# Second layer's gate and value by seven block products in place of eight, with the sums of weights and of x formed on the chip

## The chip, the cores and the metric

One core of one Trainium2 chip runs the whole program. The metric is the device time of one execution in microseconds (us); the time before is the median of three runs.

## The reference, cut to what matters

```python
def _moe_ref(x, w_in, w_out, g_ln):                 # first layer, x: 2304 x 512
    h = x @ w_in                                    # 1024 hidden
    ...                                             # softmax times h, layer norm
    return (ln @ w_out).astype(np.float32)

def _moe2_ref(x, w_gate, w_val, w_out):             # second layer
    gate = 1.0 / (1.0 + np.exp(-(x @ w_gate)))      # 512 x 1536
    val = x @ w_val                                 # 512 x 1536
    return (gate * val @ w_out).astype(np.float32)  # 1536 x 512

def reference(**kwargs):
    attn_out = _attn_ref(**attn_kwargs)             # 4 batches, 8 heads, 576 rows, 64 wide
    ...
    x = _moe_ref(x=x, **moe_kwargs)
    return _moe2_ref(x=x, **moe2_kwargs)
```

## The kernel before, in words

The program has three stages: attention over 16 pairs of heads (from the fifth pair on mixed with the first layer's tiles), the rest of the first layer alone, and the second layer. 2304 tokens are 18 tiles of 128. x lies transposed in `xT` (four rows of 128 channels by 2304 tokens). All matrix products are made from pairs of a rounded high part (`_hi`, written by ScalarE, ACT) and the remainder (`_lo`, by VectorE, DVE, or GpSimd, POOL): three matmuls (hi hi, hi lo, lo hi) for each product.

**The tail of the first layer** (the loops `for i in range(t + 1, TILES)`, t = 11, in the blocks of tensor, vector and scalar). In iteration i TensorE (PE) turns the normalized tile i (L1086, 8 transposes), turns the output of tile i-1 (L1106), makes the hidden product of tile i+2 (L1076, 24 matmuls of 512 columns) and the output product of tile i (L1099, 24 more), which waits for `ln_lo_ok`. DVE in its own order: `moe_ln_low(i)` (L821, two instructions), `moe_store_x(i-1)` (L801), the maximum of tile i+2 (L777), its rows and statistics (L784 to L812, with two trips to ACT and one to POOL), and `moe_norm` (L814). For i = 16 and 17 there is no tile i+2: in its place PE makes the first two steps of the second layer (`gate_val(0, 0)` and `(0, 1)`). Meanwhile ACT and POOL split the first 384 tokens of x (L540, L447) and the first four weight blocks (L537, L442).

**The second layer** walks over 6 chunks of 384 tokens (`CH`) and, inside one, over 12 blocks f of 128 hidden columns (`FB2`): 72 steps. A step is `gate_val(c, f)` on PE: 12 matmuls 128x384 for the gate into one bank (L1199 to L1201, 4 channel blocks by 3), 12 for the value into another; then ACT takes the sigmoid (L552), DVE multiplies by the value (L902), ACT rounds (L559), DVE subtracts (L905), and PE adds the step before into the output with `out_block` (L1214 to L1216, 3 tiles by 3 matmuls of 512 columns). After f = 11 DVE moves the three output banks out (L935) through two buffers and SyncE's queue (SP) stores them (L396). The weights are loaded once (L380 to L382), split once and stay. At a chunk's start ACT (L540) and POOL (L447, x_lo) split the next 384 tokens of x. The chunks 1 to 5 are one hardware loop on PE.

The order of work is written out by hand: each engine runs its own list, and semaphores tie them.

## Time and profile before

| | |
|---|---|
| runs | 909.24, 910.42, 910.52 us, median 910.42 |
| profiled execution | 908.74 us, its span 907.0 us |
| PE busy | 875.7 us, 97% |
| DVE, ACT, POOL busy | 407.3, 351.8, 104.4 us |
| second layer alone, 465.6 us to the end | PE without a gap but for some tenths at a chunk's start |
| moved by DMA | 33.73 MB |

The profile is of one execution. Its trace gives the start and length of each instruction, and what ended the idle time before it. A matmul's length there holds its drain: successive matmuls overlap, so what one costs is read from start to start. The span leaves out 1.7 us of the execution's time.

### The profile page before, as it was taken

The numbers are of one execution on the slowest core, as the hardware profiler recorded it, in microseconds if no ns is written. First come the engines' busy times: TensorE is split into PE (matmuls) and PEld (weight loads), VectorE is DVE, ScalarE is ACT, GpSimd is POOL, SyncE is SP. The second block draws the span as 40 slices with busy tenths as digits, with TensorE's granted clock in tenths as the row PEclk, the third lists the DMA queues.
The fourth block names the chain that finished last, engine by engine and source line by source line (L and its number), as shares of the span: only waits on it lengthen the run. The fifth ranks groups of instructions, "written<-read, shape, count | busy, mean of one in ns | idle before, by whom it ended". The sixth has DMA issues, their size and how long they took to land.

```text
span 907.0 us, 14321 instructions
## 1 busy us (share of the span) xinstructions
PE 875.7 (97%) x5440; PEld 735.8 (81%) x5440; DVE 407.3 (45%) x1104; ACT 351.8 (39%) x772; POOL 104.4 (12%) x83
## 2 busy tenths in 40 slices
PE   5788899999999999999999999999999999999997
PEld 2555677777777778778899999999999999999996
DVE  5888876766666675355425121121121112112112
ACT  4777665656665653345443121121121112112111
POOL 1000000000000001135266010010010001001000
PEclk9999999999999999999999999999999999999999
DMA  5151111111111000400350000000000000000000
GB/s 186 44 173 44 41 42 42 42 39 32 39 42 42 16 16 14 140 1 4 101 169 6 1 36 1 1 35 0 0 35 0 0 0 35 0 0 35 0 0 35
DMA packets 36803, 33.73 MB, mean 37 GB/s; under 512 B 5776, under 2 KB 27280, under 8 KB 36752
## 3 DMA queue, kind: packets, MB, share of 16 engines
q1 hardware_dynamic: 36752, 33.06, 11.8%
q8 instruction: 31, 0.51, 0.2%
q14 instruction: 20, 0.16, 0.1%
HBM read 28.33 MB, written 4.72 MB: 36 GB/s over the span
## 4 chain that ended last, share of the span: by engine, by line
PE 93%; DVE 4%; issue 1%; ACT 1%; DMA 1%; SPq 0%; POOL 0%; DVEq 0%; ACTq 0%
PE m_bk L1076 9%; PE s_bk L1099 7%; PE tt_bk L1199 6%; PE s_bk L1201 6%; PE s_bk L1199 6%; PE s_bk L1200 6%; PE tt_bk L1201 5%; PE tt_bk L1200 5%; PE o_bk L1099 4%; PE s_bk L965 4%; PE tt_bk L1013 4%; PE o_bk L1021 4%; PE m_bk L1216 4%; PE m_bk L1215 4%; PE m_bk L1214 4%; PE s_bk L1076 2%
## 5 line engine op out<-in xcount | busy, mean ns | idle before, releaser
L902 DVE TENSOR_TENSOR gv<-gv,s_bk 128x384 f32<-128x384 f32 x71 | 39.3, 554 | 279.7 <-PE s_bk L1201 279.7
L483 ACT ACTIVATE p_nat<-p_nat,negmax 128x512 f32<-128x512 f32 (+2 forms) x144 | 83.0, 578 | 75.0 <-DVE negmax L716 75.0
L552 ACT ACTIVATE gv<-tt_bk 128x384 f32<-128x384 f32 x70 | 34.5, 492 | 198.7 <-PE tt_bk L1201 198.7
L559 ACT CAST gv_hi<-gv 128x384 fp32r<-128x384 f32 x72 | 36.9, 513 | 156.6 <-PE m_bk L1216 135.9
L1199 PE MATMUL s_bk<-x_hi,w_hi 128*128 128x384 f32 x288 | 96.3, 334 | 0.0
L1201 PE MATMUL s_bk<-x_hi,w_lo 128*128 128x384 f32 x288 | 96.2, 334 | 0.0
L1200 PE MATMUL s_bk<-x_lo,w_hi 128*128 128x384 f32 x288 | 96.2, 334 | 0.0
L1199 PE MATMUL tt_bk<-x_hi,w_hi 128*128 128x384 f32 x280 | 94.8, 338 | 0.1
L1201 PE MATMUL tt_bk<-x_hi,w_lo 128*128 128x384 f32 x280 | 94.4, 337 | 0.0
L1200 PE MATMUL tt_bk<-x_lo,w_hi 128*128 128x384 f32 x280 | 94.0, 336 | 0.0
L905 DVE TENSOR_TENSOR gv_lo<-gv,gv_hi 128x384 fp32r<-128x384 f32 x72 | 51.9, 721 | 46.4 <-ACT gv_hi L559 46.4
L716 DVE CUSTOM_DVE_ANT_0 p_nat<-s_bk,mask 128x512 f32<-128x512 f32 (+3 forms) x128 | 56.5, 487 | 27.0 <-PE s_bk L965 26.8
L1013 PE MATMUL tt_bk<-ident,p_nat 128*128 128x128 f32 x400 | 56.2, 278 | 10.3 <-DVE memo L754 6.2
L1013 PEld LDWEIGHTS tt_bk<-ident,p_nat 128*128 128x128 f32 x400 | 47.1, 143 | 22.5 <-issue 16.4
L447 POOL TENSOR_TENSOR x_lo<-xT,x_hi 128x384 fp32r<-128x384 f32 x24 | 23.8, 1015 | 310.9 <-ACT x_hi L540 310.7
L965 PE MATMUL s_bk<-qkT 64*64 64x256 f32 (+3 forms) x512 | 49.6, 482 | 10.3 <-DVE negmax L716 5.7
L1216 PE MATMUL m_bk<-w_hi,gv_lo 128*128 128x512 f32 x144 | 57.1, 397 | 0.0
L1215 PE MATMUL m_bk<-w_lo,gv_hi 128*128 128x512 f32 x144 | 56.8, 395 | 0.0
L490 ACT COPY pT<-tt_bk 128x512 f32<-128x512 f32 (+1 forms) x80 | 43.1, 559 | 35.3 <-PE tt_bk L1013 33.7
L1214 PE MATMUL m_bk<-w_hi,gv_hi 128*128 128x512 f32 x144 | 56.6, 393 | 0.0
L1199 PEld LDWEIGHTS tt_bk<-x_hi,w_hi 128*128 128x128 f32 x280 | 52.6, 188 | 4.5 <-POOL x_lo L447 1.7
L1200 PEld LDWEIGHTS tt_bk<-x_lo,w_hi 128*128 128x128 f32 x280 | 52.6, 188 | 2.8
(142 smaller groups left out, 1757.5 us busy)
## 6 DMA issues: line engine op xcount, KB each, us to landing
qkT<-in_q SPq DMA_DIRECT2D x16, 288.0 KB, 2.8
qkT<-in_k SPq DMA_DIRECT2D x16, 288.0 KB, 3.2
out<-o_sb SPq DMA_DIRECT2D x18, 256.0 KB, 2.0
v_raw<-in_v SPq DMA_DIRECT2D x16, 256.0 KB, 2.7
w_raw<-in_moe_w_gate SPq DMA_DIRECT2D x12, 256.0 KB, 4.7
w_raw<-in_moe_w_val SPq DMA_DIRECT2D x12, 256.0 KB, 4.9
w_raw<-in_moe_w_out SPq DMA_DIRECT2D x12, 256.0 KB, 5.7
xT<-in_moe_w_in SPq DMA_DIRECT2D x1, 2048.0 KB, 8.5
```

Source lines behind the costliest of these rows:

```text
L483: nc.scalar.activation(p_tile(g, tile), p_tile(g, tile), ACT.Exp, bias=negmax[:, n:n + 1], scale=-1.0, accum_out=den[:, n:n + 1]).then_inc ...
L716: last = nc.vector.tensor_tensor_reduce(out=to, in0=s_tile(tile), in1=m, scale=-SCALE, scalar=3.0e38, op0=ALU.add, op1=ALU.min, accum_out= ...
L965: last = mm(s_tile(tile)[c * D:c * D + D, :], qkT[r, g % 2, 0, a:a + D], qkT[r, g % 2, 1, 0:keys(tile)], start=True, stop=True, skip_group ...
L1013: last = nc.tensor.transpose(bank[:, c * P:(c + 1) * P], p_nat[g % 2][:, p_at[tile] + j * P:p_at[tile] + (j + 1) * P], ident[:, :])
L1076: last = mm(h_banks(even)[:, n, :], x[:, b, :], w[:, b, c], start=m % (3 * DC) == 0, stop=m % (3 * DC) == 3 * DC - 1)
L1099: last = mm(y_bank(tail), ln[:, f * P:(f + 1) * P], w[:, f, :], start=m == 0, stop=m == 3 * FB - 1)
L1199: mm(o, w3_hi[f][:, a], x2_hi[:, d, :], start=d == 0, stop=False)
L1200: mm(o, w3_hi[f][:, a], x2_lo[:, d, :], start=False, stop=False)
L1201: last = mm(o, w3_lo[f][:, a], x2_hi[:, d, :], start=False, stop=d == DC - 1)
L1214: mm(o, gv_hi[b][:, t], w3_hi[f][:, w], start=f == 0, stop=False)
L1215: mm(o, gv_hi[b][:, t], w3_lo[f][:, w], start=False, stop=False)
L1216: last = mm(o, gv_lo[b][:, t], w3_hi[f][:, w], start=False, stop=f == FB2 - 1)
```

## The change

The 2304 tokens are now walked in 3 groups of 768 (two halves a and b of 384), with 12 blocks f each: 36 steps n. One step's gate and value for both halves are a product of a 2 by 2 block matrix of weights (rows gate and value, columns the two halves of the 512 channels) with a 2 by 2 block matrix of x (the halves of the channels, the halves a and b). It is made from seven block products (6 matmuls 128x384 each, two channel blocks by three):

- S1 = A21+A22, S2 = S1-A11, S3 = A11-A21, S4 = A12-S2 of the weights (A11, A12 gate; A21, A22 value), by DVE `add_w` in every step;
- T1 = B12-B11, T3 = B22-B12, T2 = B22-T1, T4 = B21-T2 of x, by DVE `add_x`, once a group;
- PE adds A11 B11, S2 T2, S1 T1, S4 B22 in this order into one bank (the chain), A12 B21, then S3 T3 and A22 T4 into the second (the side). Between them ACT copies the running sums out (`keep_p1`, `keep_u2`, `keep_u4`), and DVE adds the side to them (`gate_a`, `val_b`, `val_a`). So PE waits within a step for `p1_ok`, `gate_a_ok`, `u2_ok`, `u4_ok`, `val_b_ok`, and at the next for `sig_b_ok` and `val_a_ok`.

The six output tiles of the step before are put between the products. The gate's and value's weights are loaded and split anew in all 36 steps through three raw buffers; only the output weights stay. Their splitting and that of x goes from POOL to DVE. The loops are written out in full. The last three tiles leave through buffers of their own.

```diff
-            def split_w3(f):
-                pool.wait_ge(w3_hi_ok, f + 1)
...
-            with pool.Fori(1, CHUNKS) as c:
-                for b in range(DC):
-                    split_x2_block(c, b)
...
             def load_w3(f):
...
+                sp.dma_start(w3_raw[f][:, :], w3o_v[:, f, :]).then_inc(w3_in[f], 16)
+
+            def load_wc(n):
+                f, r = n % FB2, wc_raw[n % NR]
+                wait(sp, wc_lo_ok, 2 * (n - NR + 1))
...
             sp.wait_ge(x_ok, 2 * PAIRS)
+            load_wc(0)
+            for f in range(2):
                 load_w3(f)
             sp.wait_ge(h_ready, TILES)
+            for n in range(1, NR + 1):
+                load_wc(n)
+            sp.wait_ge(yt_ready, TILES)
+            for f in range(2, FB2):
                 load_w3(f)
...
+            for n in range(NR + 1, STEPS):
+                load_wc(n)
+                if n % FB2 == 4 and n > FB2:
+                    store_b(n // FB2 - 1)
+                    store_a(n // FB2 - 1)
```

ScalarE's list of one step (`leaves`: last f of a group, `enters`: first f of the next):

```diff
+            def pair_step(n):
...
+                keep_p1(n)
+                if leaves:
+                    split_xc(p + 1, B11)
+                sig_a(n)
+                if leaves:
+                    split_xc(p + 1, B21)
+                if enters:
+                    split_xc(p, B22)
+                keep_u2(n)
+                if enters:
+                    split_xc(p, T4)
+                if n + 1 < STEPS:
+                    split_wc(n + 1, 0)
+                    split_wc(n + 1, 1)
+                keep_u4(n)
+                if 1 < n < FB2:
+                    split_w3(n)
+                if enters:
+                    evacuate_b(p - 1)
...
+                sig_b(n)
...
+                keep_hi_b(n)
```

VectorE's list of one step, and what it does in the first layer's tail:

```diff
+            def pair_step(n):
...
+                gate_a(n)
...
+                if f == 1 and p:
+                    evacuate_a(p - 1)
+                if n == 0:
+                    add_w(1)
+                if n + 2 < STEPS and n and not enters:
+                    add_w(n + 2)
...
+                if n + 1 < STEPS:
+                    low_wc(n + 1, 0)
...
+                val_b(n)
+                if n + 1 < STEPS:
+                    low_wc(n + 1, 1)
+                if n == 0 or enters:
+                    add_w(n + 2)
+                if 1 < n < FB2:
+                    low_w3(n)
+                if 4 <= f < 8 and p < GROUPS - 1:
+                    add_x(p + 1, (T1, T3, T2, T4)[f - 4])
...
+                times_b(n)
+                val_a(n)
+                low_b(n)
+                times_a(n)
...
+                low_a(n)
...
+                if i == t + 1:
+                    dve.wait_ge(yt_ok, 2 * CT)
+                    dve.wait_ge(x_ok, 2 * PAIRS)
+                    add_x(0, T1)
+                    add_x(0, T3)
+                    add_x(0, T2)
+                    add_x(0, T4)
+                elif i == t + 2:
+                    low_xc(0, B11)
+                    low_xc(0, B21)
+                    low_xc(0, T2)
+                    low_xc(0, T3)
+                elif i == t + 3:
+                    add_w(0)
+                    low_xc(0, T1)
+                    low_xc(0, B22)
+                    low_xc(0, T4)
+                elif i == t + 4:
+                    low_w3(0)
+                    low_wc(0, 0)
+                    low_wc(0, 1)
```

TensorE's list of one step (`between(k)` is one output tile, or in steps 0 and 1 four matmuls of the first layer's output product):

```diff
+            def products(n, between):
...
+                product(n, B11, True).then_inc(chain_ready, 1)
...
+                product(n, B21, True).then_inc(side_ready, 1)
+                between(0)
...
+                pe.wait_ge(p1_ok, n + 1)
+                product(n, T2, False).then_inc(chain_ready, 1)
+                pe.wait_ge(gate_a_ok, n + 1)
+                product(n, T3, True).then_inc(side_ready, 1)
+                between(1)
+                pe.wait_ge(u2_ok, n + 1)
+                product(n, T1, False).then_inc(chain_ready, 1)
+                between(2)
+                between(3)
+                pe.wait_ge(u4_ok, n + 1)
+                product(n, B22, False).then_inc(chain_ready, 1)
+                pe.wait_ge(val_b_ok, n + 1)
+                product(n, T4, False).then_inc(side_ready, 1)
+                between(4)
+                between(5)
...
-            with pe.Fori(1, CHUNKS) as c:
-                chunk(c)
+            for n in range(2, STEPS):
+                products(n, lambda k, n=n: out_tile(n - 1, k))
+            for k in range(2 * CT):
+                out_tile(STEPS - 1, k)
```

**DVE in the first layer's tail.** Before, in iteration 14 of the tail, the norm of tile 16 (L814) is followed at once by the remainder of tile 15 (L821), for which PE's output product waits:

```order
L812 TENSOR_SCALAR st<-st 128x1
L814 TENSOR_SCALAR u_even<-u_even,st 128x1024 [waits ln_b]
L821 TENSOR_TENSOR ln_lo<-tt_bk,ln_hi 128x512 [waits ln_hi_ok] x2
L801 TENSOR_SCALAR xT<-s_bk 128x4x128 [waits yt_ready]
L777 TENSOR_REDUCE st<-m_bk 128x1 [waits h_ready]
```

Now the same place (L954 is the norm, L961 the remainder, L1062 to L1067 `add_w`, L1054 `low_xc`):

```order
L954 TENSOR_SCALAR u_even<-u_even,st 128x1024 [waits ln_b]
L1062 TENSOR_TENSOR wc_raw0<-wc_raw0 128x256 [waits wc_in0]
L1063 TENSOR_TENSOR wc_raw0<-wc_raw0 128x256
L1065 TENSOR_TENSOR wc_raw0<-wc_raw0 128x256 [waits s1_ok]
L1067 TENSOR_TENSOR wc_raw0<-wc_raw0 128x256 [waits s2_ok]
L1054 TENSOR_TENSOR xc_lo<-xc_raw,xc_hi 128x768 [waits xc_hi_ok]
L1054 TENSOR_TENSOR xc_lo<-xT,xc_hi 128x768 [waits xc_hi_ok]
L1054 TENSOR_TENSOR xc_lo<-xc_raw,xc_hi 128x768 [waits xc_hi_ok]
L961 TENSOR_TENSOR ln_lo<-tt_bk,ln_hi 128x512 [waits ln_hi_ok] x2
L941 TENSOR_SCALAR xT<-s_bk 128x4x128 [waits yt_ready]
```

Seven instructions of DVE have moved in ahead of the remainder; iterations 12, 13 and 15 have four, four and three such.

**SP's queue after the first layer.** Before (L380 gate, L381 value, L382 output weights of a block; from the wait on, five blocks of three rows):

```order
L380 DMA w_raw<-in_moe_w_gate 128x4x128
L381 DMA w_raw<-in_moe_w_val 128x4x128
L382 DMA w_raw<-in_moe_w_out 128x512
L380 DMA w_raw<-in_moe_w_gate 128x4x128 [waits yt_ready]
L381 DMA w_raw<-in_moe_w_val 128x4x128
L382 DMA w_raw<-in_moe_w_out 128x512
```

Now (L445 an output weight block, L450 and L452 value and gate of a step; the pair behind the ten blocks is `load_wc(4)`):

```order
L450 DMA wc_raw<-in_moe_w_val 128x4x128 [waits wc_lo_ok]
L452 DMA wc_raw<-in_moe_w_gate 128x4x128
L445 DMA w_raw<-in_moe_w_out 128x512 [waits yt_ready]
L445 DMA w_raw<-in_moe_w_out 128x512 x9
L450 DMA wc_raw<-in_moe_w_val 128x4x128 [waits wc_lo_ok]
L452 DMA wc_raw<-in_moe_w_gate 128x4x128
```

`load_wc(4)` stands behind ten transfers that wait for the last tile of the first layer; before, the first blocks behind that wait were those of steps 7 to 11.

## Rows read from the trace of the kernel before

**Rows 1.** The page, parts 1 and 2: PE's busy time; its granted clock in 40 slices

```profile
PE 875.7 (97%) x5440; PEld 735.8 (81%) x5440; DVE 407.3 (45%) x1104; ACT 351.8 (39%) x772; POOL 104.4 (12%) x83
...
PEclk9999999999999999999999999999999999999999
```

**Rows 2.** Busy time by stretch (stretch: length, busy us per engine, clock), second layer

```profile
600.00:700.00 100.00, 99.97 (x527) 93.26 (x527) 20.50 (x36) 17.75 (x36) 5.29 (x6) 1.00 0.04 16
```

**Rows 3.** Timeline (start, length, engine, line, operation): one step on PE

```profile
641.70 0.33 PE L1199 MATMUL tt_bk<-x_hi,w_hi 128*128 128x384 f32 x1
...
643.80 0.33 PE L1199 MATMUL s_bk<-x_hi,w_hi 128*128 128x384 f32 x1
...
645.88 0.39 PE L1214 MATMUL m_bk<-w_hi,gv_hi 128*128 128x512 f32 x1
...
647.96 0.33 PE L1199 MATMUL tt_bk<-x_hi,w_hi 128*128 128x384 f32 x1
```

**Rows 4.** Timeline of PE: the fourth step's (f = 3) first matmul

```profile
465.56 0.33 PE L1199 MATMUL tt_bk<-x_hi,w_hi 128*128 128x384 f32 x1
```

**Rows 5.** Timeline: the end, last matmul and last copy

```profile
901.62 0.40 PE L1216 MATMUL o_bk<-w_hi,gv_lo 128*128 128x512 f32 x1
903.64 0.69 DVE L935 COPY o_sb<-o_bk 128x512 f32<-128x512 f32 x1 [1.50 <-DMA out<-o_sb]
```

**Rows 6.** Groups by line and shape, DVE: subtractions of 384 (from 500 us on), 1024

```profile
L905 DVE TENSOR_TENSOR gv_lo<-gv,gv_hi 128x384 fp32r<-128x384 f32 x64 | 35.8, 560 | 40.8 <-ACT gv_hi L559 40.8
...
L766 DVE TENSOR_TENSOR w_lo<-xT,w_hi 128x1024 fp32r<-128x1024 f32 x4 | 4.9, 1216 | 0.0
```

**Rows 7.** Timeline of ACT: roundings of 384 and of 1536 columns

```profile
397.74 0.51 ACT L540 CAST x_hi<-xT 128x384 fp32r<-128x384 f32 x1
398.15 1.48 ACT L537 CAST w_hi<-w_raw 128x1536 fp32r<-128x1536 f32 x1
```

**Rows 8.** Timeline of DVE in the first layer's tail

```profile
389.25 0.81 DVE L814 TENSOR_SCALAR u_moe<-u_moe,st 128x1024 f32<-128x1024 f32 x1
...
400.15 1.29 DVE L821 TENSOR_TENSOR ln_lo<-tt_bk,ln_hi 128x512 fp32r<-128x512 f32 x2 [0.26 <-ACT ln_hi L528]
401.36 0.68 DVE L801 TENSOR_SCALAR xT<-s_bk 128x512 f32<-128x512 f32 x1
404.15 1.22 DVE L777 TENSOR_REDUCE st<-m_bk 128x1 f32<-128x1024 f32 x1 [2.12 <-PE m_bk L1076]
...
410.98 1.41 DVE L814 TENSOR_SCALAR u_moe<-u_moe,st 128x1024 f32<-128x1024 f32 x1
...
435.93 1.42 DVE L814 TENSOR_SCALAR u_moe<-u_moe,st 128x1024 f32<-128x1024 f32 x1
```

**Rows 9.** Timeline of PE there: output products of tiles 13 and 14; step 0

```profile
403.95 0.40 PE L1099 MATMUL o_bk<-w_hi,ln_hi 128*128 128x512 f32 x1
...
416.43 0.40 PE L1099 MATMUL o_bk<-w_hi,ln_hi 128*128 128x512 f32 x1
...
435.81 0.42 PE L1199 MATMUL s_bk<-x_hi,w_hi 128*128 128x384 f32 x1
```

**Rows 10.** Timeline of POOL there: the split of x

```profile
410.82 1.02 POOL L447 TENSOR_TENSOR x_lo<-xT,x_hi 128x384 fp32r<-128x384 f32 x1 [0.25 <-ACT x_hi L540]
```

**Rows 11.** Timeline of SP's queue, and busy time by stretch (last number GB/s)

```profile
461.62 0.37 SPq L380 DMA_DIRECT2D w_raw<-in_moe_w_gate  x1
...
471.84 1.25 SPq L382 DMA_DIRECT2D w_raw<-in_moe_w_out  x1
...
476.00:478.00 2.00, 2.00 (x11) 1.65 (x10) 1.14 (x2) 0.51 (x1) 1.93 (x1) 1.00 0.22 77
```

**Rows 12.** Busy time by stretch (granted clock third from the end), early attention

```profile
24.00:26.00 2.00, 1.10 (x7) 0.83 (x7) 0.68 (x4) 1.91 (x6) 0.00 (x0) 0.87 0.06 10
26.00:28.00 2.00, 1.80 (x8) 1.35 (x7) 1.24 (x5) 0.73 (x3) 0.00 (x0) 0.50 0.03 8
28.00:30.00 2.00, 1.87 (x13) 1.19 (x12) 1.94 (x3) 1.58 (x6) 0.00 (x0) 0.78 0.00 0
```

More of the change, by code:

```diff
@@ L82, in attn_moe_kernel @@
     T_END = PAIRS - M0
+    A22, A11, A12, S1, S2, S3, S4 = range(7)
+    B11, B21, T2, T3, T1, B22, T4 = range(7)
+    W_OF = (A11, A12, S2, S3, S1, S4, A22)
+    SIDE = (0, 1, 0, 1, 0, 0, 1)
+    STEPS = GROUPS * FB2
+    OUT_TILES = (3, 4, 5, 0, 1, 2)
     with ExitStack() as ctx:
@@ L389, in _ @@
+            sp.wait_ge(yt_ready, TILES)
+            for f in range(2, FB2):
                 load_w3(f)
[L390 to L401 removed]
@@ new lines, in split_xc @@
+            def split_xc(p, j):
+                if p:
+                    n = p * FB2 - 1
+                    if SIDE[j]:
+                        act.wait_ge(side_ready, 3 * n + (B21, T3, T4).index(j) + 1)
+                    else:
+                        act.wait_ge(chain_ready, 4 * n + (B11, T2, T1, B22).index(j) + 1)
+                if j in (T1, T2, T3, T4):
+                    act.wait_ge(xs_ok, 4 * p + (T1, T3, T2, T4).index(j) + 1)
+                elif p == 0:
+                    act.wait_ge(yt_ok, 2 * CT)
+                nc.scalar.copy(xc_hi[:, j, :, :], x_sum(p, j)).then_inc(xc_hi_ok, 1)
@@ new lines, in keep_p1, with sig_a, keep_u2 @@
+            def keep_p1(n):
+                act.wait_ge(chain_ready, 4 * n + 1)
+                nc.scalar.copy(c_p1[:, :], pair_banks(n)[0]).then_inc(p1_ok, 1)
+            def sig_a(n):
+                act.wait_ge(gate_a_ok, n + 1)
+                wait(act, lo_a_ok, n)
+                nc.scalar.activation(gv_a[:, :], c_p1[:, :], ACT.Sigmoid).then_inc(sig_a_ok, 1)
+            def keep_u2(n):
+                act.wait_ge(chain_ready, 4 * n + 2)
+                wait(act, gv_a_ok, n)
+                nc.scalar.copy(c_u2[:, :], pair_banks(n)[0]).then_inc(u2_ok, 1)
@@ new lines, in keep_u4, with sig_b, keep_hi_b @@
+            def keep_u4(n):
+                act.wait_ge(chain_ready, 4 * n + 3)
+                wait(act, gv_b_ok, n)
+                nc.scalar.copy(c_u4[:, :], pair_banks(n)[0]).then_inc(u4_ok, 1)
+            def sig_b(n):
+                act.wait_ge(chain_ready, 4 * n + 4)
+                wait(act, lo_b_ok, n)
+                nc.scalar.activation(gv_b[:, :], pair_banks(n)[0], ACT.Sigmoid).then_inc(sig_b_ok, 1)
+            def keep_hi_b(n):
+                act.wait_ge(gv_b_ok, n + 1)
+                wait(act, out_ready, 2 * CT * (n - 2) + CT if n > 1 else 0)
+                nc.scalar.copy(gv_hi[1][n % 2][:, :], gv_b[:, :]).then_inc(hi_b_ok, 1)
@@ new lines, in pair_step @@
+            def pair_step(n):
+                p, f = n // FB2, n % FB2
+                enters, leaves = f == 0 and p > 0, f == FB2 - 1 and p < GROUPS - 1
+                gate_a(n)
+                if leaves:
+                    low_xc(p + 1, B11)
+                if enters:
+                    low_xc(p, T1)
+                    low_xc(p, B22)
+                if f == 1 and p:
[4 more added lines that the diff above has]
+                    add_w(n + 2)
+                if leaves:
+                    low_xc(p + 1, B21)
+                if n + 1 < STEPS:
+                    low_wc(n + 1, 0)
+                if enters:
+                    low_xc(p, T4)
+                val_b(n)
[7 more added lines that the diff above has]
+                    add_x(p + 1, (T1, T3, T2, T4)[f - 4])
+                if leaves:
+                    low_xc(p + 1, T2)
+                times_b(n)
+                val_a(n)
+                low_b(n)
+                times_a(n)
+                if leaves:
+                    low_xc(p + 1, T3)
+                low_a(n)
```

487 lines of the change are left out of this document (293 added, 194 removed).

## The prediction

> **What bounds the kernel now.** I read the page first: PE is busy 97% of the span at full clock [rows 1]. Then the busy times by stretch: in the second layer PE is busy 99.97 of 100 us, DVE 20.5 and ACT 17.8 [rows 2]. Then the timeline of one step on PE. The gate takes 643.80-641.70 = 2.10 us, the value 2.08, the output block 2.08, and the next step follows at once: 6.26 us in all [rows 3]. So a matmul of 384 columns costs 2.08/12 = 0.173 us, one of 512 columns 2.08/9 = 0.231, and the first product behind an output block some 0.02 more. From 465.56 [rows 4] PE runs to 901.62+0.23 = 901.85 [rows 5], 436.3 us. The work in it, 69 gates and values of 4.18 and 70 output blocks of 2.08, is 434.0; the other 2.3 us are the starts of five chunks. PE's columns are the limit, so fewer of them are worth their time wherever PE needn't wait for something new.
>
> **What is removed.** Per block f and 768 tokens there were 48 matmuls of 384 columns, now 42; the 18 of 512 stay. Two old steps take 12.52 us. A new one: 42 x 0.173 = 7.28, 18 x 0.231 = 4.16, four returns from an output tile to a product 0.08, together 11.52. Over 36 steps **-36.0**. The chunk starts go with the chunks: **-2.3**; what stands in their place is costed below. At the end, 907.0-901.85 = 5.15 us lie behind PE, since the third copy had to wait for a store [rows 5]. Now each last tile has its own buffer: 0.1 + copy 0.69 + store (907.0-903.64-0.69 = 2.67) = 3.5. **-1.7**. The gain without any new wait is 40.0.
>
> **The steady step, by its queues.** Prices: two-input DVE instructions of 384 columns 0.56, of 1024 1.22 [rows 6], so by the line between them 256 take 0.43 and 768 0.95 (0.08 less from start to start). ACT roundings: 384 take 0.51, 1536 1.48 [rows 7], so 768 0.83 and 1024 1.05. DVE has per step 7 of 384 (3.9), `add_w` 4 x 0.43 = 1.7 with its own waits, `low_wc` 0.95+1.22: 7.8 us of 11.5. ACT has 7 x 0.5 + 0.83 + 1.05 = 5.4. Neither binds by its sum. By order, from the step's start: B11 ends at 1.04, B21 2.08, T2 runs 2.77 to 3.81, T3 to 4.85, T1 5.54 to 6.58, B22 7.97 to 9.01, T4 to 10.05 (about 0.2 more until a result may be read).
> - `keep_p1` 1.2 to 1.75 is in time for T2 at 2.77. `gate_a` 2.3 to 2.9 is in time for T3 at 3.81.
> - `keep_u2` 4.0 to 4.5, for T1 at 5.54. Behind it on ACT the two splits end at 6.4, so `keep_u4` runs 6.8 to 7.3, for B22 at 7.97: the tightest, 0.65 us over.
> - `val_b` 7.3 to 7.9 for T4 at 9.01. `sig_b` and `times_b` end at 10.3, `val_a` 10.9, for B21 of the next step at 12.56. `low_a` ends at 1.7 of the next step, before `gate_a`.
> In steps 4 to 11 `low_w3` (0.7) and an `add_x` (0.95) stand ahead of `times_b`, which comes at 10.7: still in time. I take no wait; `add_w`, `low_wc` and the splits are hidden under PE's products, and if that cover fails they cost what rival 4 prices. The reload of 512 KB per step is hidden too: a buffer comes free some 17 us before it is wanted, and transfers have landed within the 14.9 us that 15 of them took [rows 11].
>
> **The first layer's tail: +7.2.** Here DVE's additions stand ahead of what PE waits for. Before, the remainder of tile 13 (L821) ends at 401.44 and PE wants it at 403.95: 2.5 us of slack [rows 8, 9]. The old splits on POOL go, which had held the norm at 1.41 us while POOL split x [rows 8, 10]; alone it takes 0.81, so 0.6 comes back in each iteration.
> - Iteration 12: four `add_x`, 3.6 us, less 2.5 and 0.6, is 0.5. But ACT's split of T2 waits for the third sum and holds its own rounding of tile 13: 0.8.
> - From then on DVE is the longer ring: maximum to norm's end 412.39-404.15 = 8.24, less 0.6, then the addition, the remainder 1.45, the store of x 0.6: 9.7 plus the addition, against PE's 12.48 (416.43-403.95). Iteration 13 adds four `low_xc`, 3.6: +0.8. Iteration 14 adds `add_w(0)` 1.7 and three `low_xc` 2.65: +1.5.
> - Step 0 on PE was due at 435.81, now 438.9. It waits for `low_wc(0, 0)`. The norm of tile 17 ended at 437.35; now 0.6 sooner and 3.4 later, at 440.15, then `low_w3(0)` and `low_wc(0, 0)` until 441.7: +2.85.
> - The remainder of tile 16 behind `low_wc(0, 1)`: +0.4. In iteration 17 the turn of tile 16's output waits for ACT, whose copy now stands behind both halves of step 0: +0.8.
> Sum 7.15. Ends: 0, if the idle time of DVE took it all, and 14, which is all that DVE is given there (14.4).
>
> **Step 2: +3.8.** Step 2 starts where 465.56 was, plus 2.0 (twelve matmuls more are due by then) plus 7.2: 474.8; the last tile of x is turned at 472.0. That frees ten output-weight transfers, and `load_wc(4)` stands behind them. Before, 15 transfers of 256 KB took from 461.62 to about 476.5 [rows 11]. Twelve then take 11.9 and some 0.6 to be seen: 484.5. DVE comes to `add_w(4)` at 477.7 and sits; behind it are `low_wc(3, 0)` and `val_b(2)`, which end at 487.6. PE wants `val_b` at 474.8+9.0 = 483.8. Ends: 0 and 8 (if the transfers of 512-byte rows at the end go at half the rate). The Trainium skill, in "DMA: Bandwidth & Descriptors", section "Anatomy of one DMA", gives a fit of 2.0 us plus bytes by 436 GB/s, measured on another path. By it the twelve would be there after 9.2 us, the wait would be 0.5 and the sum 3.3 us lower; the rows of this queue (3.93 MB in 14.9 us, 264 GB/s) speak against it.
>
> **Group entries: +2.** In steps 11, 12 and 13 DVE gets seven `low_xc` and three copies, ACT seven splits and three copies. By the same lists `keep_u4(12)` is 0.2 late and `gate_a(13)` 0.1 to 0.3; with latencies 1 us for each of two entries. Ends 0 and 3 each, the latter if one list goes wholly late.
>
> **Sum.** 907.0-40.0+7.2+3.8+2.0 = 880.0 for the span, 1.7 more for the profiled execution (908.74 before), and the median before lies 1.7 over that execution (910.42): **883.5**.
>
> **Rivals.**
> 1. Nearly smooth: DVE's idle time takes the tail's additions and the queue keeps up. For it: DVE idles 2.1 us before each maximum [rows 8]. Against it: the additions stand behind the norm, not in that gap. Losses of 3: 873.5.
> 2. The clock falls. In early attention, in a stretch where PE was busy 1.10 of 2 us and then again little, the granted clock went to 0.87, 0.50 and 0.78 in three slices, so down to 1.2 GHz, which cost (0.13+0.50+0.22) x 2 = 1.7 us [rows 12]. The waits of 2.85 at step 0 and 3.8 at step 2 are such idle times: +3.4, 887. The Trainium skill, "TensorE: Matmul & The Clock Gate", section on the clock gate, makes the slow clock the default that only sustained work lifts; by it both waits would be followed by slow matmuls, and the trace agrees for attention.
> 3. A heavy start: DVE's and ACT's lists in the tail hold each other up (as T2's split does) to the upper end, and step 2 waits its 8: losses of 25, 895.
> 4. Slower: the ring between PE, ACT and DVE binds in each step. Place: `keep_u4` behind both splits on ACT, then `val_b`. It decides from 0.65 us of lateness there; to use up the 26.9 us, all of 34 steps must wait 0.8, so the two splits and the copy must take 1.45 more than 2.4. Each further 0.3 costs 10 us: 920 at 2.0. For it: five waits a step that were not there. Against it: every price comes from rows of the same shape, and DVE and ACT are quiet [rows 2].
>
> **How the numbers follow.** My sum 0.45, rival 1 0.13, rival 2 0.2, rival 3 0.14, rival 4 0.08 (a little of it not slower). About 0.2% (1.8 us) is what a measurement of this kernel can tell from none. Faster 0.92, within 0.2% 0.02, slower 0.06. Range: 873 to 898 leaves out the far part of rivals 1 and 3 and most of 4.
>
> **What would show it.** In the profile after: PE's period in steps 14 to 22 is 11.5 us, and PE waits there for nothing; if it is above 12, rival 4. PE waits for L961's remainder in iterations 13 to 15, some 3 us, and for L1073 before its first product of the second layer. In step 2 one wait of 3 to 5 us for L1089, DVE itself idle at L1062 on the DMA. The granted clock after these two waits tells rival 2. The last matmul is 3.5 us before the end. I am wrong in the main if the second layer's steps are not even, or if PE's matmul of 384 columns no longer goes at 0.173.

## The result, and the profile after

The changed kernel takes **880.54 us** (median of four runs, 878.8 to 883.05) against 910.42: ratio 0.9674, 95% interval 0.9659 to 0.969. The forecast was 883.5, the range 873 to 898. The profiled execution took 881.66 us, its span 879.7.

PE stays the bound, with 96% of a shorter span. DVE and ACT took over work: in the second layer DVE is now busy 70.7 of 100 us and ACT 47.1, where before it was 20.5 and 17.8 [rows 2]. From the page and the busy times by stretch (stretch: length, busy us of PE, PEld (its weight loads), DVE, ACT, POOL with counts, granted clock, DMA share, GB/s) of the changed kernel:

```profile
PE 842.2 (96%) x5224; PEld 700.8 (80%) x5224; DVE 601.7 (68%) x1464; ACT 464.2 (53%) x958; POOL 38.2 (4%) x47
...
600.00:700.00 100.00, 100.00 (x522) 92.86 (x521) 70.71 (x124) 47.11 (x83) 0.00 (x0) 1.00 0.20 63
```

The first matmuls of three steps in PE's timeline (start, length) give the period: 653.57 - 642.07 = 11.50 us, and over the steps 3 to 11 it is 11.48 or 11.49. The step that enters the second group (from 595.96) is hardly longer: the three steps around it take 11.52, 11.53 and 11.58.

```profile
595.96 0.33 PE L1449 MATMUL tt_bk<-xc_hi,wc_hi 128*128 128x384 f32 x1
...
642.07 0.34 PE L1449 MATMUL tt_bk<-xc_hi,wc_hi 128*128 128x384 f32 x1
...
653.57 0.34 PE L1449 MATMUL tt_bk<-xc_hi,wc_hi 128*128 128x384 f32 x1
```

**The tail**, to be held against [rows 8, 9]: the norm alone takes 0.81, four additions of 0.95 (the last two start 1.0 apart) stand ahead of the remainder L961, and PE waits behind it (the last bracket of a row is the idle time before it and what ended it).

```profile
400.30 0.81 DVE L954 TENSOR_SCALAR u_even<-u_even,st 128x1024 f32<-128x1024 f32 x1
401.03 0.95 DVE L1042 TENSOR_TENSOR xc_raw<-xT 128x768 f32<-128x768 f32 x1
...
405.10 1.29 DVE L961 TENSOR_TENSOR ln_lo<-tt_bk,ln_hi 128x512 fp32r<-128x512 f32 x2 [0.39 <-ACT ln_hi L596]
```

```profile
406.49 0.48 PE L1356 MATMUL o_bk<-w_hi,ln_hi 128*128 128x512 f32 x1 [0.67 <-issue]
...
442.35 0.41 PE L1449 MATMUL s_bk<-xc_hi,wc_hi 128*128 128x384 f32 x1 [2.36 <-issue]
```

**Step 2**, in three timelines. SP issues ten output-weight blocks and then the two transfers of `load_wc(4)`; DVE stands at L1062 until the second of them has landed, 7.74 us; PE stands behind DVE's L1089, 4.26 us.

```profile
472.32 5.85 SPq L445 DMA_DIRECT2D w_raw<-in_moe_w_out  x10
478.22 0.43 SPq L450 DMA_DIRECT2D wc_raw<-in_moe_w_val  x1
478.69 0.51 SPq L452 DMA_DIRECT2D wc_raw<-in_moe_w_gate  x1
479.24 0.73 SPq L450 DMA_DIRECT2D wc_raw<-in_moe_w_val  x1
```

```profile
485.53 0.42 DVE L1062 TENSOR_TENSOR wc_raw<-wc_raw 128x256 f32<-128x256 f32 x1 [7.74 <-DMA wc_raw<-in_moe_w_gate]
...
487.87 0.55 DVE L1089 TENSOR_TENSOR c_u<-c_u,tt_bk 128x384 f32<-128x384 f32 x1
```

```profile
488.47 0.44 PE L1449 MATMUL tt_bk<-xc_hi,wc_hi 128*128 128x384 f32 x1 [4.26 <-DVE c_u L1089]
```

Behind that wait the granted clock (third number from the end) falls. The burst of transfers starts slowly, at 76 and 177 GB/s in its first two slices; ahead of PE's wait the DMA engines are full (share 0.99 and more) at 318 to 353 GB/s.

```profile
472.00:474.00 2.00, 2.00 (x12) 1.65 (x11) 0.69 (x1) 0.00 (x0) 0.00 (x0) 1.00 0.31 76
474.00:476.00 2.00, 2.00 (x12) 1.82 (x11) 0.00 (x0) 0.00 (x0) 0.00 (x0) 1.00 0.63 177
...
480.00:482.00 2.00, 2.00 (x12) 1.82 (x11) 0.00 (x0) 1.36 (x3) 0.00 (x0) 1.00 0.99 318
482.00:484.00 2.00, 2.00 (x12) 1.67 (x10) 0.00 (x0) 0.80 (x2) 0.00 (x0) 1.00 1.11 353
...
488.00:490.00 2.00, 1.53 (x6) 1.53 (x7) 2.00 (x3) 0.00 (x0) 0.00 (x0) 0.76 0.00 0
490.00:492.00 2.00, 2.00 (x6) 1.61 (x6) 1.89 (x5) 0.51 (x1) 0.00 (x0) 0.50 0.56 168
492.00:494.00 2.00, 2.00 (x11) 1.86 (x11) 0.79 (x2) 0.69 (x2) 0.00 (x0) 0.88 0.32 94
```

**The end**, PE's and DVE's timelines, against [rows 5]: 879.7 - 876.23 = 3.5 us behind the last matmul, where 5.15 lay.

```profile
876.00 0.39 PE L1502 MATMUL s_bk<-w_hi,gv_loa 128*128 128x512 f32 x1
```

```profile
876.43 0.69 DVE L1123 COPY wc_raw<-s_bk 128x512 f32<-128x512 f32 x1
```

**How executions are compared.** The two spans differ by 27.3 us, but attention, whose code is the same, ended 1.7 us later in this execution: the hidden product behind it starts at 386.92, before at 385.21. So each trace is also read from that product to the end of its span, and called its rest: 907.0 - 385.21 = 521.8 us before, 879.7 - 386.92 = 492.8 after. The difference is 29.0. All twelve runs by both measures, each ratio against runs of the kernel before on the same chip. The variants ran on several chips, so two of them are compared by their ratios, not by their medians:

| kernel | time, us (runs) | ratio, interval | hidden product at | rest, us |
|---|---|---|---|---|
| before | 910.42 (4) | 1 | 385.21 | 521.8 |
| changed | 880.54 (4) | 0.9674, 0.9659 to 0.969 | 386.92 | 492.8 |
| e5_again, the same | 880.67 (5) | 0.9676, 0.9662 to 0.9689 | 385.84 | 492.7 |
| e1_queue | 877.06 (5) | 0.9636, 0.9619 to 0.9654 | 385.64 | 486.9 |
| e2_eight | 878.85 (5) | 0.9657, 0.9639 to 0.9675 | 386.94 | 491.5 |
| e3_slots | 881.34 (5) | 0.9676, 0.9654 to 0.9698 | 386.83 | 492.5 |
| e4_both | 875.68 (5) | 0.9614, 0.9598 to 0.9629 | 387.01 | 486.9 |
| e6_slots2 | 879.72 (5) | 0.966, 0.9647 to 0.9673 | 388.00 | 489.5 |
| e7_both2 | 873.16 (5) | 0.9584, 0.957 to 0.9599 | 386.76 | 484.4 |
| e9_best | 872.27 (5) | 0.9587, 0.9574 to 0.96 | 386.82 | 483.4 |
| e8_eighth | 917.8 (1) | none | 388.18 | 527.6 |
| e10_act2 | 883.18 (2) | 0.9703, 0.9685 to 0.9722 | 385.66 | 494.9 |
| e11_act4 | 895.8 (2) | 0.9842, 0.9823 to 0.9861 | 388.05 | 506.6 |
| e12_dve2 | 882.42 (2) | 0.9695, 0.9676 to 0.9714 | 386.70 | 492.9 |

### The profile page after: what moved, and what is told of

It reads as the page before. It is cut to its first block, busy times and chain, and to the rows that moved or that the text cites. A ratio compares the mean times of both kernels' runs of the same rounds, so it can differ in the third digit from the quotient of the medians.

```text
span 879.7 us, 14380 instructions
## 1 busy us (share of the span) xinstructions
PE 842.2 (96%) x5224; PEld 700.8 (80%) x5224; DVE 601.7 (68%) x1464; ACT 464.2 (53%) x958; POOL 38.2 (4%) x47
## 4 chain that ended last, share of the span: by engine, by line
PE 90%; DVE 5%; issue 2%; DMA 1%; ACT 1%; SPq 1%; POOL 0%; DVEq 0%; ACTq 0%
PE m_bk L1333 10%; PE tt_bk L1449 9%; PE tt_bk L1451 9%; PE tt_bk L1450 9%; PE s_bk L1356 7%; PE tt_bk L1270 5%; PE s_bk L1222 4%; PE o_bk L1356 4%; PE o_bk L1278 4%; PE s_bk L1501 3%; PE s_bk L1500 3%; PE s_bk L1502 3%; PE s_bk L1250 2%; PE s_bk L1333 2%; PE m_bk L1501 2%
## 5 line engine op out<-in xcount | busy, mean ns | idle before, releaser
L1449 PE MATMUL tt_bk<-xc_hi,wc_hi 128*128 128x384 f32 x476 | 160.1, 336 | 4.3 <-DVE c_u L1089 4.3
L1451 PE MATMUL tt_bk<-xc_hi,wc_lo 128*128 128x384 f32 x476 | 160.2, 337 | 0.0
L1450 PE MATMUL tt_bk<-xc_lo,wc_hi 128*128 128x384 f32 x476 | 160.0, 336 | 0.0
L1073 DVE TENSOR_TENSOR wc_lo<-wc_raw,wc_hi 128x768 fp32r<-128x768 f32 x72 | 78.3, 1088 | 30.8 <-ACT wc_hi L616 30.8
L1449 PEld LDWEIGHTS tt_bk<-xc_hi,wc_hi 128*128 128x128 f32 x476 | 89.5, 188 | 10.8 <-DVE c_u L1089 4.6
L1450 PEld LDWEIGHTS tt_bk<-xc_lo,wc_hi 128*128 128x128 f32 x476 | 89.5, 188 | 6.1
L1451 PEld LDWEIGHTS tt_bk<-xc_hi,wc_lo 128*128 128x128 f32 x476 | 89.5, 188 | 0.0
L616 ACT CAST wc_hi<-wc_raw 128x768 fp32r<-128x768 f32 x72 | 64.5, 945 | 1.8 <-DVE wc_raw L1067 1.8
L1333 PE MATMUL m_bk<-w_hi,x_hi 128*128 128x512 f32 x120 | 50.3, 419 | 1.5 <-issue 1.3
L880 DVE TENSOR_SCALAR p_nat<-p_nat,c_loc 128x512 f32<-128x512 f32 (+2 forms) x144 | 49.1, 398 | 1.7
L1333 PE MATMUL m_bk<-w_hi,x_lo 128*128 128x512 f32 x120 | 47.1, 393 | 0.0
L1089 DVE TENSOR_TENSOR c_u<-c_u,tt_bk 128x384 f32<-128x384 f32 x34 | 18.8, 554 | 36.1 <-ACT c_u L648 36.1
```

Of the source, the lines that this page charges most:

```text
L616: nc.scalar.copy(wc_hi[n % 2][:, k, :, :], wc_raw[n % NR][:, r, :, :]).then_inc(wc_hi_ok, 1)
L880: nc.vector.tensor_scalar(p, p, c_loc[:, t:t + 1], None, ALU.mult).then_inc(p_ok, 1)
L1073: nc.vector.tensor_tensor(wc_lo[n % 2][:, k, :, :], wc_raw[n % NR][:, r, :, :], wc_hi[n % 2][:, k, :, :].bitcast(F32), ALU.subtract).then_ ...
L1333: last = mm(h_banks(even)[:, n, :], x[:, b, :], w[:, b, c], start=m % (3 * DC) == 0, stop=m % (3 * DC) == 3 * DC - 1)
L1449: mm(o, hi[:, k, c, :], xc_hi[:, j, c, :], start=start and c == 0, stop=False, skip_group_check=True)
L1450: mm(o, hi[:, k, c, :], xc_lo[:, j, c, :], start=False, stop=False, skip_group_check=True)
```

## The experiments

### Do PE's columns set the period?

**e8_eighth**: one more block product in each step.

```diff
-                product(n, B22, False).then_inc(chain_ready, 1)
+                product(n, B22, False)
+                product(n, B22, False).then_inc(chain_ready, 1)
```

> Edit: TensorE makes the product S4 B22 twice in each step (eight block products in place of seven, nothing else), so the gate of half b holds it twice. My theory (TensorE's columns set the period: 6 matmuls of 0.173 us more): the period goes from 11.49 to 12.53 us, the time rises by 37.4 us to about 918. Rival (the period of 11.49 is set by the ring through ScalarE and VectorE, with TensorE's columns close below it): less than 30 us.

The period became 12.53 us (+1.04, six matmuls at 0.173), and a stretch of 100 us is full with matmuls again. (Its output is not the reference's, since the product is added twice.) The rest grew by 34.8 us. 36 x 1.04 = 37.4; the remaining -2.6 lie in step 2, where the wait was 3.17 in place of 4.26 and the clock did not fall (below). So a product of six matmuls costs just what it occupies on PE, and -36 for the removed ones is no accident. It is one execution, but the 1.04 us stand in each of its steady steps.

### How near are the other engines?

**e10_act2** and **e11_act4**: two and four more copies on ACT ahead of `keep_u4`.

```diff
+                if n > 1:
+                    for k in range(4):
+                        wait(act, pad_ok, 4 * (n - 2) + k - 1)
+                        nc.scalar.copy((pad0, pad1)[k % 2][:, 0:CH], c_p1[:, :]).then_inc(pad_ok, 1)
                 keep_u4(n)
```

> Edit: the changed kernel with two more ScalarE copies of 384 columns ahead of keep_u4 in steps 2 to 35. In a steady step of the profile ScalarE idles 0.62 us before keep_u4, and the copy is over 0.71 us before the product B22 that waits for it: 1.33 us, less some 0.1 for the semaphore. My theory: two copies (0.9 us) are hidden, period 11.49 us, hidden product to end 492.8 us. Rival (the period is already set by this ring): +0.9 us a step, +30 us.

> Edit: four such copies (1.7 to 1.8 us). My theory (the ring of TensorE and ScalarE binds from 1.2 us of addition on): 0.5 to 0.6 us of them show in each of 34 steps, period 12.0 to 12.1, +17 to +20 us (time 898 to 901), with TensorE waiting for keep_u4 before B22 in every step. Rival (more hidden, since what is late in one step is taken up in the next): under 5 us.

With two copies the period stays at 11.49; only the steps that enter a group take 0.5 and 0.3 more. The rest grew by 2.2, of which 1.3 are a fall of the clock in step 0 (below) and 0.8 these entries. With four the period is 11.85 to 11.94, 0.36 to 0.45 over, and the steps that enter a group take 13.27 and 12.67; the rest grew by 13.8, less than the 17 expected. In ACT's timeline of one step of e11_act4 (and PE's below it) the four copies come without a gap, then `keep_u4`, then B22:

```profile
643.37 1.75 ACT L693 COPY pad<-c_p 128x384 f32<-128x384 f32 x4
...
645.03 0.47 ACT L649 COPY c_u<-tt_bk 128x384 f32<-128x384 f32 x1
```

```profile
645.55 0.45 PE L1454 MATMUL tt_bk<-xc_hi,wc_hi 128*128 128x384 f32 x1
```

`keep_u4` starts 645.03-643.37 = 1.66 us behind the first copy. Of those 1.66 some 0.4 show, so about 1.3 are hidden. That agrees with the changed kernel's own rows (ACT's, then PE's): ACT idles 0.62 us before `keep_u4`, and the copy's end, 648.90+0.48 = 649.38, is 0.71 ahead of the B22 product at 650.09.

```profile
648.90 0.48 ACT L648 COPY c_u<-tt_bk 128x384 f32<-128x384 f32 x1 [0.62 <-PE tt_bk L1451]
```

```profile
650.09 0.33 PE L1449 MATMUL tt_bk<-xc_hi,wc_hi 128*128 128x384 f32 x1
```

**e12_dve2**: two more additions on DVE in steps 4 to 35.

```diff
                     add_w(n + 2)
+                if 3 < n:
+                    nc.vector.tensor_tensor(pad1[:, :], w3_lo[2][:, :].bitcast(F32),
+                                            w3_lo[2][:, :].bitcast(F32), ALU.add)
+                    nc.vector.tensor_tensor(pad0[:, 0:CH], w3_lo[2][:, 0:CH].bitcast(F32),
+                                            w3_lo[2][:, 0:CH].bitcast(F32), ALU.add)
```

> Edit: the changed kernel with two more VectorE additions (512 and 384 columns, some 1.1 us) behind add_w(n+2) in steps 4 to 35. VectorE idles 0.97 us before low_wc(n+1, 0) and 1.17 before val_b. My theory: hidden, period 11.49, no change (492.8 us from hidden product to end), but some tenths in the steps that enter a group. Rival (VectorE, busy 71 of 100 us in the second layer, is the bound behind TensorE): +1.1 us in 32 steps, +35 us.

Hidden: period 11.49, rest 492.9, with 0.1 and 0.4 us in the two steps at the first group entry. DVE is now busy 79.4 of 100 us there, and PE doesn't notice. Rival 4 (the ring binds) is out: on ACT about 1.3 us of work find room in a steady step, on DVE at least the 1.1 tried here.

### The wait in step 2

**e1_queue**: step 4's weights are asked for before the ten output-weight blocks.

```diff
-            for n in range(1, NR + 1):
+            for n in range(1, NR + 2):
                 load_wc(n)
...
-            for n in range(NR + 1, STEPS):
+            for n in range(NR + 2, STEPS):
                 load_wc(n)
```

> Edit: the weights of step 4 are asked for right after those of step 3, ahead of the ten output-weight transfers. My theory (step 2 waits because its VectorE list stands at add_w(4) for a transfer that is queued behind those ten; the fallen clock after it is the wait's consequence): TensorE's wait of 4.3 us for L1089 goes, the granted clock stays at 1.00 from 485 to 495 us, step 2 takes 11.5 us in place of 17.6, and the time falls by 6 us to about 874.5. Rival (the transfers are only moved: the ten output-weight blocks land later, so low_w3(2) and the output products of step 2 or 3 wait in its place): steps 2 to 4 together lose 3 us or more, 877 to 880. Rival (the clock falls there for another reason than the wait): slices below 1.00 remain near 490 us, 876.3.

What the theory said of step 2 holds to a tenth; both rivals are out. SP issues the pair of L450 and L452 at 450.98, DVE goes through L1062 without a wait, step 2 takes 485.20-473.66 = 11.54 us and step 3 11.59 (no loss moved there), and the clock is 1.00 throughout. From the trace of this variant, PE's timeline, DVE's timeline, and the busy times where the wait had been:

```profile
473.66 0.34 PE L1449 MATMUL tt_bk<-xc_hi,wc_hi 128*128 128x384 f32 x1
...
485.20 0.34 PE L1449 MATMUL tt_bk<-xc_hi,wc_hi 128*128 128x384 f32 x1
```

```profile
476.44 0.42 DVE L1062 TENSOR_TENSOR wc_raw<-wc_raw 128x256 f32<-128x256 f32 x1
```

```profile
484.00:488.00 4.00, 4.00 (x21) 3.64 (x21) 2.63 (x6) 1.51 (x3) 0.00 (x0) 1.00 0.43 129
```

The rest fell by 5.9 us, the 6 of the theory, but the median is 877.06 and not 874.5. By the ratios the gain is (0.9674 - 0.9636) x 910 = 3.5 us, and the intervals of the two ratios allow some 2 more or less. The same edit on the two variants with other places gives (0.9676 - 0.9614) x 910 = 5.6 and (0.966 - 0.9584) x 910 = 6.9. The three average 5.3.

**e2_eight**: step 4's weights after eight of the ten blocks.

```diff
-            for f in range(2, FB2):
+            for f in range(2, 10):
                 load_w3(f)
+            load_wc(NR + 1)
+            for f in range(10, FB2):
+                load_w3(f)
```

> Edit: the weights of step 4 are asked for after eight of the ten output-weight transfers. My theory (twelve transfers of 256 KB took some 13 us, about 1 us each, and what stands ahead in the queue is what is waited for): they land some 2 us sooner, TensorE's wait in step 2 falls from 4.3 to about 2.3 us. The clock tells how long a wait it bears: it fell behind 4.3 us and not behind 2.36 us at step 0. If it stays at 1.00 behind 2.3 us, the time falls by 2.0+1.8 = 3.8 us to 876.7; if any such wait in step 2 lets it fall, by 2.0 to 878.5.

The wait is 2.99 us, 1.3 shorter and not 2, and the clock falls as before; the rest is 1.3 lower. DVE goes through L1062 1.3 us sooner. SP issues the pair at 477.12 and 477.60, then the last two blocks and step 5's pair. The packets say in which order they move: a step's weights go in packets of 512 bytes, 1024 for a pair, and an output-weight block in packets of 2 KB. The DMA view of this variant counts, from 472 to 481, 481 to 483, 483 to 484 and 484 to 487.5 us:

```profile
DMA packets 1148, 2.09 MB, mean 232 GB/s; under 512 B 118, under 2 KB 142, under 8 KB 1147
DMA packets 1090, 0.65 MB, mean 325 GB/s; under 512 B 41, under 2 KB 1017, under 8 KB 1090
DMA packets 226, 0.37 MB, mean 372 GB/s; under 512 B 19, under 2 KB 53, under 8 KB 226
DMA packets 1089, 0.58 MB, mean 165 GB/s; under 512 B 46, under 2 KB 1060, under 8 KB 1089
```

Of 512 bytes ("under 2 KB" less "under 512 B") these are 24, 976, 34 and 1014. So step 4's pair moves mostly between 481 and 483, the last two blocks mostly behind it, and step 5's pair last: the order of issue, with an overlap of under 1 us. That what is issued behind a transfer slows it is not shown. What was mispriced is the block: at the 318 to 353 GB/s of the full slices 256 KB take 0.74 to 0.82 us, and 1 us is the mean with the slow start. Two blocks are then 1.5 to 1.6 us; why the gain is 1.3 stays open.

### The tail

**e3_slots**: the same additions and remainders, in places where DVE was thought idle (the three lists of an iteration: before the maximum, before the rows, before the variance; a fourth, from e6_slots2 on, behind the norm).

```diff
+            SLOTS = {
+                t + 1: ([(first_sum, 0, T1), (add_x, 0, T3)], [(add_x, 0, T2)], [(add_x, 0, T4)]),
+                t + 2: ([(low_xc, 0, B11), (low_xc, 0, B21)], [(low_xc, 0, T2)], [(add_w, 0)]),
+                t + 3: ([(low_xc, 0, T3), (low_xc, 0, T1)], [(low_xc, 0, B22)], [(low_xc, 0, T4)]),
+                t + 4: ([(low_w3, 0), (low_wc, 0, 0)], [(low_wc, 0, 1)], []),
+            }
```

> Edit: in the first layer's tail VectorE does the same additions and remainders of the second layer's operands, but in its idle places (before the maximum of tile i+2, before its rows, before its variance) and not behind the norm, ahead of the remainder that TensorE waits for. My theory (the 5.6 us that the tail takes longer come from the place of the additions, since VectorE idles 2 us before each maximum and in its trips to ScalarE): the tail costs 0 to 1.5 us, step 0 starts 50.6 to 52 us after the hidden product at 386.9 in place of 55.4, and the time falls by 4 to 5 us to about 876. Rival (VectorE's ring is full by its sum, and the place doesn't matter): the maximum or the rows come later by as much, the tail keeps its 5 us, 880.

No gain: step 0 starts 442.49-386.83 = 55.7 us behind the hidden product (55.4 in the changed kernel). The rival (a full ring, so the place doesn't matter) seems right by the time, and for iteration 12 it is. There DVE has no idle time before the maximum, and the first addition runs beside POOL's work in 1.98 us in place of 0.95; the maximum comes 2.8 us later, and PE waits 2.70 for a copy of ACT behind it. Behind that wait the granted clock falls as well, (0.30+0.50+0.05) x 2 = 1.7 us in three slices: from the output product of tile 12 to that of tile 13 PE takes 409.92-392.97 = 16.95 us, where it took 12.59 before the change, 4.4 more. POOL's, DVE's and PE's timelines of this variant, and its busy times by stretch:

```profile
393.26 1.29 POOL L509 TENSOR_TENSOR x_lo<-xT,x_hi 128x512 fp32r<-128x512 f32 x1 [2.81 <-ACT x_hi L579]
```

```profile
393.38 1.98 DVE L1042 TENSOR_TENSOR xc_raw<-xT 128x768 f32<-128x768 f32 x1
395.29 0.94 DVE L1044 TENSOR_TENSOR xc_raw<-xT 128x768 f32<-128x768 f32 x1
396.15 1.21 DVE L917 TENSOR_REDUCE st<-s_bk 128x1 f32<-128x1024 f32 x1
```

```profile
402.37 0.41 PE L1362 MATMUL s_bk<-ident,y_nat 128*128 128x128 f32 x2 [2.70 <-ACT y_nat L601]
```

```profile
402.00:404.00 2.00, 1.63 (x7) 1.47 (x8) 1.15 (x3) 2.00 (x4) 0.55 (x1) 0.70 0.03 8
404.00:406.00 2.00, 2.00 (x6) 1.52 (x6) 1.06 (x2) 1.40 (x3) 0.00 (x0) 0.50 0.00 0
406.00:408.00 2.00, 2.00 (x10) 1.62 (x9) 2.00 (x4) 0.00 (x0) 0.00 (x0) 0.95 0.00 0
```

From iteration 13 on the loss was gone but for 0.6 us in iteration 14 (where PE waits 0.47 for ACT's copy): step 0 starts 442.49-435.58 = 6.91 us behind the output product of tile 15, as before the change (435.81-428.90), where the changed kernel takes 9.62.

**e4_both**: this with the queue's edit.

> Edit: both the earlier request for step 4's weights and the additions in VectorE's idle places. My theory (the two losses are separate, one ring in the first layer's tail, one queue in step 2): the gains add, 6+5 = 11 us, about 869.5, and TensorE waits for nothing of note from 387 us on. Rival (they are not separate: a tail that ends 5 us sooner wants the transfers of the queue 5 us sooner): less than the sum, 872 to 875.

Rest 486.9, the same as the queue's edit alone: one gain of 5.9 and one of nothing add. The 11 us of the theory needed the gain that e3_slots didn't bring, so its rival is not decided here. Iteration 12 lost the same here, a wait of 2.70 and a fallen clock behind it.

**e6_slots2**: nothing before the maximum in iteration 12 (the diff is against e3_slots; ACT's splits of T2 and T4 come one iteration later too).

```diff
-                t + 1: ([(first_sum, 0, T1), (add_x, 0, T3)], [(add_x, 0, T2)], [(add_x, 0, T4)]),
+                t + 1: ([], [(first_sum, 0, T1)], [(add_x, 0, T3)], []),
+                t + 2: ([(add_x, 0, T2), (low_xc, 0, B11)], [(add_x, 0, T4)], [(low_xc, 0, B21)], []),
...
+                t + 4: ([(low_xc, 0, B22), (low_xc, 0, T4)], [(low_w3, 0)], [(low_wc, 0, 0)], [(low_wc, 0, 1)]),
```

> Edit: VectorE's additions in its idle places, but none before the maximum in iteration 12, where it has no idle time (there the trace of the first such variant shows the additions ending 2.8 us after the maximum could begin, and TensorE waiting 2.70 us for the copy that ScalarE makes behind it); two of the four sums of x move to iteration 13, and ScalarE's split of T2 with them. My theory (the loss of the tail is where the additions stand): step 0 starts 50.6 to 51.6 us after the hidden product in place of 55.4, the time from hidden product to end falls from 492.8 to about 488.4, and the time by 4 us. Rival (the ring of the tail is full by its sum and any place costs): again 55 us and no gain.

Step 0 now starts 439.89-388.00 = 51.9 us behind the hidden product, 3.5 sooner and 0.3 short of the forecast; in DVE's timeline the addition fits between maximum and rows:

```profile
394.56 1.22 DVE L917 TENSOR_REDUCE st<-s_bk 128x1 f32<-128x1024 f32 x1
395.69 0.95 DVE L1042 TENSOR_TENSOR xc_raw<-xT 128x768 f32<-128x768 f32 x1
397.05 1.22 DVE L924 CUSTOM_DVE_ANT_0 u_even<-e_moe,s_bk 128x1024 f32<-128x1024 f32 x1 [0.41 <-ACT e_moe L583]
```

A new wait, in PE's timeline, takes 1.1 us back within step 0, since `low_wc(0, 1)` stands ahead of the remainder of tile 16:

```profile
443.36 0.47 PE L1356 MATMUL o_bk<-w_hi,ln_hi 128*128 128x512 f32 x1 [1.11 <-issue]
```

The rest fell by 3.3 in place of 4.4 (two waits of 0.5 for ACT's copy, L1363, are new as well). The ratios, (0.9676 - 0.966) x 910 = 1.5 us apart, can't tell it from nothing nor from 3.3.

**e7_both2**: both edits.

> Edit: the same places and step 4's weights asked for before the ten output-weight transfers. My theory: the gains add, 5.9+4.4 us from hidden product to end (492.8 to 482.5), the time about 870. Rival (with a tail 4.4 us shorter the transfers behind the last tile of x are late: output weights of block 2 or 3, wanted in steps 3 and 4): 1 to 3 us of it come back as a wait for L1078 or in step 3.

Rest 484.4, 8.3 below the changed kernel: 5.9+3.3 less 0.9, since the step 2 that starts sooner had already a shorter wait (3.40) in the variant without the queue's edit. By the ratios, 0.9584 and 0.9674, it is 8.2 us below the changed kernel too. The rival's late output weights don't show.

**e9_best**: the remainder of tile 16 first (the diff is against e7_both2).

```diff
-                t + 4: ([(low_xc, 0, B22), (low_xc, 0, T4)], [(low_w3, 0)], [(low_wc, 0, 0)], [(low_wc, 0, 1)]),
+                t + 4: ([(low_xc, 0, B22), (low_xc, 0, T4)], [(low_w3, 0)], [(low_wc, 0, 0)], []),
...
                 moe_ln_low(i)
+                if i == t + 5:
+                    low_wc(0, 1)
                 moe_store_x(i - 1)
```

> Edit: as the kernel with both changes of place and queue (ratio 0.9584), and in iteration 16 VectorE makes the remainder of tile 16 before the second half of step 0's weights, not behind it. My theory (the 1.11 us for which TensorE waits in step 0 behind L961 come from low_wc(0, 1) ahead of it): the wait shrinks to 0.1 us, the weights' half is ready 0.3 us late at most, and hidden product to end takes 483.5 to 484 in place of 484.4; the time about 872.3. Rival: T2's product waits for the half as long, no gain.

The wait is gone and the rest 483.4, 1.1 lower. The time, 872.27 us, can't be told from that of e7_both2 (ratios 0.9587 and 0.9584). These two are the fastest, some 38 us below the kernel before the change.

### Once more the same kernel

**e5_again**:

> Edit: none, the changed kernel once more, on the chip of the three that follow. The 1.7 us by which the hidden product at 386.9 us came later than before (385.2) lie in attention, whose code is the same; in five traces of the changed kernel and its variants it starts at 385.6 to 387.0. My theory (this part varies from execution to execution, and the rest doesn't): the hidden product again starts between 385 and 387.5, from it to the end of the span 492.8 us +-0.3 pass again, and the wait in step 2 is again 4.3 us with a fallen clock behind it. Rival (the landing in step 2 varies as well): a wait there that differs by over 1 us, and another rest.

The rest is 492.7 against 492.8, the wait 4.15 against 4.26, the clock falls again; the hidden product starts at 385.84 in place of 386.92. So it is attention that differs between these two executions, not what follows it.

## Why the prediction held, and where its terms were off

The rest was forecast to change by -36.0-2.3-1.7+7.2+3.8+2.0 = -27.0; it changed by -29.0. Attention took 1.7 back in the profiled execution, and the span came out at 879.7 for 880.0. That is nearer than the terms deserve. The median, 880.54, lies 3.0 under the forecast for another reason: it is 1.1 us below the profiled execution (881.66), and the forecast had put it 1.7 above, as it was before the change. The terms one by one:

- **Removed matmuls, -36.0 and chunk starts -2.3.** Right; e8_eighth shows the price of the matmuls, the chunk starts are borne out only by the sum. The period is 11.48 to 11.49 and not 11.52: 36 x 0.03, about -1.1 more. Matmuls of 384 columns still go at 0.173.
- **The end, -1.7.** Right (3.5 us).
- **The tail, +7.2.** Measured 5.6: step 2 starts 474.93-386.92 = 88.0 us behind the hidden product; before, [rows 4], 465.56+2.0-385.21 = 82.4. By pieces, from the starts of the output products: 0.83 (0.8 forecast), 0.34 (0.8), 0.95 (1.5), step 0 9.62-6.91 = 2.7 (2.85), and 0.8 for the last two together (0.4+0.8). The first three pieces are 2.1 of the 3.1 forecast, and PE's rows show 0.67 and 0.69 us of waiting for the remainder in iterations 13 and 15 and none of note in 14, where some 3 were to be seen. The mechanism (the place behind the norm) is shown by e3 and e6 together, for 3.5 of the 5.6. The sentence "DVE idles 2.1 us before each maximum" was wrong for iteration 12 (in the trace before the change too the maximum at 391.77 follows the store of x at once), and e3_slots, which rested on it, failed there.
- **Step 2, +3.8.** The wait was 4.3, the chain of causes as forecast (e1_queue removes all of it). The landing, forecast at 484.5, came at 485.5: the burst began 0.3 later, at 472.32, and took 13.2 us until DVE went on, not 12.5. The mean rate of the forecast held. By the DMA view's counts, until 485.5 the ten blocks and 1688 packets of 512 bytes had moved, 3.49 MB in 13.2 us, 264 GB/s. What was wrong is the count: 664 of these packets are more than step 4's pair has, so a good half of step 5's pair, issued from 479.24 on, moved before step 4's was seen. Whether it held that one up is not shown. The 436 GB/s of the Trainium skill, "DMA: Bandwidth & Descriptors", section "Anatomy of one DMA", is above what any slice of 2 us of this burst shows, and the wait of 0.5 that follows from it is not what the trace has.
- **Group entries, +2.0.** Measured 0.16 each. The step that failed is "`keep_u4(12)` is 0.2 late": it ended 0.6 us early (602.90+0.47 against B22 at 603.96 in the profile after). I had added ACT's durations, but where its instructions stand back to back each starts some 0.1 us before the one ahead ends, and five of them make half a microsecond of the 0.8 by which the forecast missed; the rest is not traced. The prediction had taken such a distance into account for DVE (0.08), and not for ACT.
- **Rival 2 (the clock falls)** came half true and was left out of the sum. Behind the wait in step 2 it fell, (0.24+0.50+0.12) x 2 = 1.7 us, the price that [rows 12] gave; behind the wait of 2.36 at step 0 it stayed at 1.00. The two terms that were too large (tail 1.6, entries 1.7) and the period (1.1) paid for this 1.7, the 0.5 of the longer wait and attention's 1.7.
- **Rivals 1, 3 and 4.** Losses were 5.6+6.1+0.3 = 12, neither 3 nor 25. Rival 4's margin was forecast at 0.65 us of lateness; the trace has 0.71, and e11_act4 needed about 1.3 us of work, 0.6 of it in ACT's idle time. In rival 4's own prices there is a slip: at 10 us for each 0.3 beyond 1.45, 920 belongs to about 1.75 and 2.0 gives about 929.

## What to carry to other kernels

When products are removed at the price of sums on other engines, the saved matmuls count in full as long as each engine's list keeps a margin at its tightest hand-over; read that margin as idle time before the instruction plus the time to its user, from distances between starts, not from sums of lengths. The losses sit at the seams, where the new operands must first come into being: look there for the engine's idle places iteration by iteration, since a place that is idle in one iteration is full in the next. And ask for the weights that the first steps want before a burst that nobody waits for: here the queue moved what it was given in the order of issue.
